# One ACT copy for both heads' transposed probabilities, from two neighbouring PSUM banks, in a fused attention, dense and expert kernel

## What is computed

```python
B, H, S, D = 4, 8, 576, 64
stride = 32
scores = (1.0 / np.sqrt(D)) * np.matmul(q, k.transpose(0, 1, 3, 2))
rel = pos[:, None] - pos[None, :]
mask_local = (rel >= 0) & (rel < stride)
mask_strided = (rel >= 0) & (pos[None, :] % stride == pos[:, None] % stride)
# heads 0-3 take mask_local, heads 4-7 mask_strided
scores = np.where(masks, scores, -1e9)
attn = np.exp(scores - scores.max(-1)); attn = attn / (attn.sum(-1) + 1e-9)
out = np.matmul(attn, v)
```

## Time and profile before

| what | us |
|---|---|
| median of 3 runs | 921.23 |
| lowest and highest | 920.25 to 929.77 |
| the profiled execution | 919.86 |
| its span, first to last instruction | 918.1 |
| PE busy in the span | 827.4 (90%) |
| ACT busy in the span | 459.6 (50%) |

### The profile page before, as it was taken

The page is one execution under the profiler, slowest core; times in us unless marked ns, Lnnn a source line. Parts: engine busy times, 40 slices in busy tenths (PEclk is TensorE's granted clock), DMA queues, the critical chain, the costliest instruction groups (busy, mean ns, idle before and its releaser), DMA issues. The chain is left out here.

```text
span 918.1 us, 17021 instructions
## 1 busy us (share of the span) xinstructions
PE 827.4 (90%) x6075; PEld 735.1 (80%) x6075; DVE 582.6 (63%) x1463; ACT 459.6 (50%) x1073; POOL 209.1 (23%) x258
## 2 busy tenths in 40 slices
PE   6878779999998999999999997249799999999995
PEld 4656568889988999999999996248688888889994
DVE  4668648768765786786686665657566666663111
ACT  5889757555554554555555452022235253353561
POOL 7910201322421152151242110010120111202211
PEclk8789879999998999999999999559799999999998
DMA  7866623555565456556645442177486595967960
GB/s 247 294 203 207 211 90 93 188 201 191 201 218 175 149 194 226 187 184 227 209 161 190 164 138 81 46 258 265 149 305 220 201 340 184 315 231 234 367 215 26
DMA packets 74198, 183.19 MB, mean 200 GB/s; under 512 B 7056, under 2 KB 26512, under 8 KB 74128
## 3 DMA queue, kind: packets, MB, share of 16 engines
q1 hardware_dynamic: 50176, 96.97, 30.7%
q0 software_dynamic: 23808, 84.95, 27.6%
q10 hardware_dynamic: 144, 0.31, 0.1%
HBM read 134.50 MB, written 47.71 MB: 198 GB/s over the span
## 5 line engine op out<-in xcount | busy, mean ns | idle before, releaser
L772 ACT ACTIVATE d_angle<-d_angle 128x384 f32<-128x384 f32 x96 | 50.6, 527 | 167.8 <-DVE d_angle L700 167.8
L642 PE MATMUL d_x<-k_w_hi,d_gl 128*128 128x512 f32 x288 | 115.3, 400 | 2.5 <-issue 2.5
L641 PE MATMUL d_x<-k_w_hi,d_gh 128*128 128x512 f32 x288 | 115.0, 399 | 0.7 <-DVE d_gl L710 0.6
L643 PE MATMUL d_x<-k_w_lo,d_gh 128*128 128x512 f32 x288 | 114.6, 398 | 0.0
L696 DVE TENSOR_SCALAR d_turns<-d_h 128x384 int32<-128x384 f32 x96 | 53.3, 556 | 82.7 <-PE d_h L624 82.7
L579 POOL DMA_DIRECT2D w_low<-k_raw x64 | 36.4, 569 | 267.7 <-DVE k_raw L740 267.7
L710 DVE TENSOR_TENSOR d_gl<-d_angle,d_gh 128x384 fp32r<-128x384 f32 x96 | 68.6, 714 | 32.0 <-ACT d_gh L781 28.3
L624 PE MATMUL d_h<-k_xh,k_w_hi 128*128 128x384 f32 x384 | 84.5, 343 | 1.7 <-PEq L130 1.7
L624 PE MATMUL d_h<-k_xh,k_w_lo 128*128 128x384 f32 x384 | 84.3, 342 | 0.0
L624 PE MATMUL d_h<-k_xl,k_w_hi 128*128 128x384 f32 x384 | 83.4, 340 | 0.0
L740 DVE TENSOR_TENSOR k_raw<-k_raw,d_high 128x1024 fp32r<-128x1024 f32 x64 | 78.1, 1220 | 0.0
(11 more groups left out here) (190 smaller groups left out, 1813.8 us busy)
## 6 DMA issues: line engine op xcount, KB each, us to landing
k_raw<-in_w POOLq DMA_DIRECT2D x64, 512.0 KB, 5.1
w_low<-k_raw POOLq DMA_DIRECT2D x64, 512.0 KB, 3.0
k_raw<-in_w SPq DMA_DIRECT2D x64, 512.0 KB
k_w_lo<-w_low SPq DMA_DIRECT2D x64, 512.0 KB, 5.5
a_v<-in_vW SPq DMA_DIRECT2D x16, 384.0 KB, 3.2
a_q<-in_qT SPq DMA_DIRECT2D x16, 288.0 KB, 3.9
x<-k_plain SPq DMA_DIRECT2D x16, 288.0 KB, 3.3
k_xl<-x SPq DMA_DIRECT2D x6, 768.0 KB, 7.8
```

Of the source, the lines that this page charges most:

```text
L641: nc.tensor.matmul(ps_x[m][:], gh[f % GR][:, g], wh[1][:, w], start=f == 0, stop=False)
L642: nc.tensor.matmul(ps_x[m][:], gl[f % GR][:, g], wh[1][:, w], start=False, stop=False)
L643: last = nc.tensor.matmul(ps_x[m][:], gh[f % GR][:, g], wl[1][:, w], start=False, stop=f == FC - 1)
L772: nc.scalar.activation(angle[i][:], angle[i][:], ACT.Abs).then_inc(s_abs, 1)
```

## The change

The two transposed banks become one tensor of two neighbouring banks, one per head. PE transposes both units of a group in one go, in the even slot, behind `attend`. ACT copies both banks with one instruction, in the odd slot, in front of the exponentials (LAG_COPY = 3, so that slot j takes units j-3 and j-2). The copy in the even slot is gone. `s_ptcopy` counts groups. The normalised probabilities have four buffers in place of two, and the copied ones two of double size in place of four.

```diff
-        probs2, bias2, total2, recip2 = (
+        probs = [sb(f"probs{i}", [P, TQ, P], f32) for i in range(PROBS)]      # PROBS = 4
+        bias2, total2, recip2 = (
...
-        pt4 = [sb(f"pt{i}", [P, TQ * STR_Q], f32) for i in range(PTS)]
+        pt2 = [sb(f"pt{i}", [P, 2, TQ * STR_Q], f32) for i in range(2)]
...
-        ps_t2 = [pb(f"probsT{i}", [P, 512]) for i in range(2)]
+        ps_t = pb("probsT", [P, 2, 512])
...
-        LAG_NORM, LAG_T, LAG_PV, LAG_OUT, MAX_LAG = 1, 2, 4, 5, 5
+        LAG_NORM, LAG_T, LAG_COPY, LAG_PV, LAG_OUT, MAX_LAG = 1, 2, 3, 4, 5, 5
...
             def transposes(b, x):
-                j = x % UNITS
-                w, kw = kind(j)
-                pe.wait_ge(s_norm, UNITS * b + x + 1 + SCORES)
-                pe.wait_ge(s_ptcopy, UNITS * b + x + 1)
-                for t in range(TQ):
-                    last = nc.tensor.transpose(ps_t2[j % 2][0:kw, t * w:(t + 1) * w], probs2[j % 2][0:w, t, 0:kw],
-                                               identf[0:w, 0:w])
-                last.then_inc(s_pt, 1)
+                w, kw = kind(x % UNITS)
+                pe.wait_ge(s_ptcopy, GROUPS * b + x // 2)
+                for h in range(2):
+                    pe.wait_ge(s_norm, UNITS * b + x + h + 1 + SCORES)
+                    for t in range(TQ):
+                        last = nc.tensor.transpose(ps_t[0:kw, h, t * w:(t + 1) * w],
+                                                   probs[(x + h) % PROBS][0:w, t, 0:kw], identf[0:w, 0:w])
+                    last.then_inc(s_pt, 1)
...
             def attend(b, x):
-                pe.wait_ge(s_ptcopy, UNITS * b + x + 2 + SEED)
+                pe.wait_ge(s_ptcopy, GROUPS * b + x // 2 + 1)
...
             def slot(b, j, run):                                   # PE
-                if run(0) and j % 2 == 0:
+                if j % 2:
+                    return
+                if run(0):
                     scores(b, j)
+                if run(LAG_PV):
+                    attend(b, j - LAG_PV)
                 if run(LAG_T):
                     transposes(b, j - LAG_T)
-                if run(LAG_PV) and j % 2 == 0:
-                    attend(b, j - LAG_PV)
...
             def copy_transposed(b, x):
-                act.wait_ge(s_pt, UNITS * b + x + 1 + SEED)
-                if not (isinstance(b, int) and b == 0 and x < PTS):
-                    act.wait_ge(s_pv, UNITS * b + x + 1 - PTS + SEED)
-                nc.scalar.activation(pt4[j % PTS][0:kw, 0:TQ * w], ps_t2[j % 2][0:kw, 0:TQ * w], ACT.Copy)\
+                act.wait_ge(s_pt, UNITS * b + x + 2 + PROBS)
+                if not (isinstance(b, int) and b == 0 and x < 4):
+                    act.wait_ge(s_pv, UNITS * b + x - 2 + SEED)
+                nc.scalar.activation(pt2[j // 2 % 2][0:kw, :, 0:TQ * w], ps_t[0:kw, :, 0:TQ * w], ACT.Copy)\
                     .then_inc(s_ptcopy, 1)
...
             def slot(b, j, run):                                   # ACT
-                if run(LAG_T):
-                    copy_transposed(b, j - LAG_T)
+                if run(LAG_COPY) and j % 2 == 1:
+                    copy_transposed(b, j - LAG_COPY)
```

More of the change, by code:

```diff
@@ L42 @@
 SEED, DMA_SEED = 2, 16
-PTS, VCOLS = 4, 4 * TQ * D
+PROBS = 4
 INV2PI = 0.15915494309189535
@@ L135, in attention @@
         v = [sb(f"v{i}", [P, 2, 2 * TQ, D], f32) for i in range(2)]
-        probs2, bias2, total2, recip2 = (
+        probs = [sb(f"probs{i}", [P, TQ, P], f32) for i in range(PROBS)]
+        bias2, total2, recip2 = (
             [sb(f"{name}{i}", shape, f32) for i in range(2)] for name, shape in (
-                ("probs", [P, TQ, P]), ("bias", [P, TQ]), ("total", [P, TQ]), ("recip", [P, TQ])))
-        pt4 = [sb(f"pt{i}", [P, TQ * STR_Q], f32) for i in range(PTS)]
+                ("bias", [P, TQ]), ("total", [P, TQ]), ("recip", [P, TQ])))
+        pt2 = [sb(f"pt{i}", [P, 2, TQ * STR_Q], f32) for i in range(2)]
         x02 = [plain[:, S * i:S * (i + 1)] for i in range(2)]
@@ L279, in stream @@
                 slot(B, j, lambda lag, j=j: j < lag)
-        LAG_NORM, LAG_T, LAG_PV, LAG_OUT, MAX_LAG = 1, 2, 4, 5, 5
+        LAG_NORM, LAG_T, LAG_COPY, LAG_PV, LAG_OUT, MAX_LAG = 1, 2, 3, 4, 5, 5
         @block.tensor
         def _(pe):
-            pe.sem_inc(s_pt, SEED)
+            pe.sem_inc(s_pt, PROBS)
             pe.sem_inc(s_pv, SEED)
@@ L335, in attend @@
                                                 v[i][0:kw, h, TQ * half + t, :],
-                                                pt4[(j + h) % PTS][0:kw, t * w + skip:(t + 1) * w],
+                                                pt2[j // 2 % 2][0:kw, h, t * w + skip:(t + 1) * w],
                                                 start=t == 0, stop=t == TQ - 1)
@@ L387, in normalise @@
                 dve.wait_ge(s_pt, UNITS * b + x + 1)
-                nc.vector.tensor_tensor(probs2[i][0:w, :, 0:kw], sv,
+                nc.vector.tensor_tensor(probs[x % PROBS][0:w, :, 0:kw], sv,
                                         recip2[i][0:w, :].unsqueeze(2).to_broadcast([w, TQ, kw]),
@@ L405, in _ @@
         def _(act):
-            act.sem_inc(s_ptcopy, SEED)
             act.sem_inc(s_x0, SEED)
```

## The result

The changed kernel takes 913.72 us (median of 5 runs, 909.92 to 918.31) against 922.66 us for the kernel before in the same comparison: a ratio of 0.989 with a 95% interval of 0.984 to 0.994. That is about 1% faster and outside the predicted range of 917 to 932 us. The profiled execution took 909.92 us.

A forecast was written before the change was run, and what follows sets the result against it. Attention was taken as bound by ACT, in balance with the DVE and PE chain, at the high clock and by PE at the low; 4.6 - 2.1 + 0.3 = +2.8 us gave 924.0 us, range 917 to 932.

The forecast's parts named there:

- Faster by over 1%: Whole kernel: outcome given 0.05, needing three clock falls to stay away and shorter stalls too.
- the second sentence of the prediction: Dense stage: starts at the program's block boundary, so it shifts by attention's gain or loss, which can be computed alone.
- Low-clock groups: Attention at the low clock: PE bounds each group at 4.44 us and the new order costs nothing.
- rival B: Attention: longer groups shrink k waits, so clock falls stay away; -3.3 us for one, -6.6 for two; chance 0.12.
- The group: Attention at the high clock: each group of two units takes 3.50 us in place of 3.28, +0.22.
- the 0.29 us of idle behind DVE's bias: ACT before even units' exponentials: without the copy ACT idles 0.25 to 0.3 us, so removing it gives only 0.03.
- the merged copy: ACT's odd slot: the doubled copy costs about 0.25 us more, 0.65 to 0.75 us in all.
- the single pair of banks: PE's transposes: one pair of probsT banks instead of two costs nothing, with a margin of 0.2 us.
- Shorter waits for k: PE's mask matmuls in attention: longer groups shorten three long k waits and remove two small ones, -2.1 us.
- the copy that fills a wait: ACT's even slot: the copy costing 0.41 us fills an existing wait, so removing it saves only 0.03 us a group.
- +4.6 us for the groups: Attention: 21 high-clock groups, each 0.22 us longer; low end 0 to -0.6, high end +8.2.

The follow-up runs named there:

- e10: The kernel before without TensorE's redundant wait on s_ptcopy in front of odd units' transposes; 916.20 us against 920.92.
- e9: The changed kernel with each TensorE wait on s_norm in front of transposes written twice; 920.66 us against 920.92 for the kernel before.
- e13: Same kernel as e10 (the kernel before without the odd units' redundant wait), measured again; 913.34 us against 922.23 for the kernel before.
- e1: The changed kernel with its merged copy split into two, one per bank, both in the odd slot; 913.96 us against 921.60 for the kernel before.
- e5: The kernel before with TensorE's new order alone, ACT copying in every slot as before; 925.58 us against 922.96.
- e8: The changed kernel as it is, measured again; 912.68 us against 922.96 for the kernel before.
- e14: The changed kernel as it is, measured once more; 909.82 us against 922.23 for the kernel before.
- e2: The kernel before with one extra small ACT copy in front of attended in each odd slot; 922.09 us against 921.60.
- e6: The changed kernel with TensorE's old order, one merged copy in the odd slot; 919.11 us against 922.96 for the kernel before.
- e7: The kernel before with only ACT's even-slot copy moved into the odd slot, as two single copies; 925.50 us against 922.96.
- e12: The kernel before as it is, a single run for a second trace; 922.43 us.
- e15: The kernel before without the odd units' redundant wait and with q and k loaded earlier; 897.94 us against 922.23 for the kernel before.
- e16: The changed kernel with q and k loaded earlier; 906.99 us against 922.23 for the kernel before.
- e11: Same kernel as e15 (q and k loaded earlier, redundant wait left out), in an earlier round; 899.09 us, ratio to the kernel before 0.971 to 0.984.
- e3: The kernel before with q and k loads issued earlier on SP, ahead of the previous pair's v load and store; 905.73 us against 921.60.

## Why the prediction was wrong, and where it was right

The forecast had the sign wrong: +2.8 us, measured -9. Faster by over 1% was given 0.05, and it is what the ratio of 0.989 says, if by a hair; its interval reaches from 0.984 to 0.994.

**The step that failed first** is the second sentence of the prediction: "whatever attention gains or loses moves everything behind it by the same amount". It held for the data and the semaphores. It did not hold for the code. Twenty-one fewer instructions on TensorE moved the dense loop, and with it went the idle time at its first turn and the instruction packets. That took 4.8 us off the dense stage in the two traces; by the medians of whole runs the place of the code is worth 4.7 us (e10 against the kernel before), 7 us (e9 against the changed kernel) or 8.9 us (e13 against the kernel before). The row was in the trace of the kernel before, 2.54 us of "issue" at 289.95 us, and so were the q8 packets; the prediction looked at neither.

**The second was the count of low-clock groups.** "Low-clock groups ... Cost nothing" took as given that as many groups stay at the low clock. The length of the spells inside attention (before the drain), by the granted clock of each trace, in us:

```
TensorE's new order:  change 13.6   e1 13.7   e5 13.6   e8 13.6   e14 10.2   e9 17.0
TensorE's old order:  before 34.1   e2 34.1   e6 34.1   e7 34.1   e12 20.5   e13 23.9   e10 6.8
```

With the old order the spells are longer in six traces of seven. Each trace is one execution, and e10 and e13, which are the same kernel, have 6.8 and 23.9. Where the clock rose before 11 us, the sums include a first spell of 3.4 or 6.8 us around 13 us, in the fill; without it 10.2 to 17.0 us stand against 20.5 to 34.1, and e10's 6.8. The longest spell is that of e6, from 30 to 57 us with PE busy throughout:

```profile
30.00:57.00 27.00, 27.00 (x191) 20.23 (x192) 15.68 (x59) 18.68 (x77) 18.83 (x35) 0.50 0.70 233
```

TensorE is busy throughout in the 3.4 us spells of the changed kernel as well, and does the same matmuls; with the new order, attend and six transposes stand in one run. Whether that is why the clock comes back sooner was not settled by any run: e10 shows that the old order can be spared too. The new order alone makes the even slot's copy wait (e5, 13.6 us of spells and no gain), and the copies in the odd slot alone lengthen the group (e7); the two parts gain, if at all, together. This was rival B in kind, given 0.12, and priced at -3.3 or -6.6 for spells that stay away. It came true in part, by shorter spells and not by the longer groups that the prediction named: e7 has the longer groups and gained nothing.

**What held.** The group: 3.49 us for 3.50 forecast, the 0.29 us of idle behind DVE's bias, the merged copy at 0.657 and 0.744 us for 0.66 and 0.73 (0.417 + 0.24, 0.464 + 0.27). No wait of the transposes for the single pair of banks. Shorter waits for k (5.5 us for 8.4, forecast 6.3). The argument itself, the copy that fills a wait, shows in e7, where only the copy is moved (+0.18 us a group), and in e15 and e16, where neither waits for k nor the idle time in dense stand beside it: +9.1 us, of which about 6 by this term. In the kernel as it is, the term was outweighed. For the two profiled executions I estimate: +4.6 us for the groups, as forecast; 5.5 - 8.4 = -2.9 for the waits for k; and for 34.1 - 13.6 = 20.5 us less at the low clock, where a group takes 4.44 us in place of 3.50, -4.3. That makes -2.6, where attention measured -3.3. The dense stage adds -4.8, and the last -1.8 lies within the spread of the rest of the span. Against e12's 20.5 us of spells the gain by the clock is only some 1.5 us, so this term differs much from one execution to the next.

The fastest version is neither kernel: e11 and e15, the old attention with q and k loaded earlier and the redundant waits left out, at 897.9 to 899.1 us, 22 to 24 us under the kernel before.

## What to carry to other kernels

Before an edit to one stage is called harmless for the next, look for "issue" rows such as the one of 2.54 us here at a loop's start and for instruction packets inside a loop: then the number of instructions ahead of it can be part of the timing, and a test with waits that never wait tells this apart from the change itself. An instruction that fills a wait is free, so taking it away and lengthening another one is a loss even on an engine that is 98% busy (e7). Where a DMA wait is followed by a low clock, remove the wait first: here it was worth 16 us (e3), and it turned the sign of the other change round.

## What the runs showed that was not expected

The dense loop runs without any code fetch for over 120 us, or with one packet of 16 KB about every 24 us (5 in 120), by 16 to 21 instructions more or less ahead of it; the stall comes near the first turn of the loop, 2.5 to 4.6 us. The place that decides lies between 406 (e10, none) and 422 (before, stall). A wait for k of 1.20 us was followed by a low-clock spell of 27 us (e6, the wait before 29.37 us), one of 1.53 us by none (the changed kernel, before 27.85 us).
